# Attention of a fused kernel: transposes, projections and codes of the next head placed one by one between a group's other blocks

## The reference

```python
q_bits = (np.einsum('bhsd,dk->bhsk', q, proj) > 0)
k_bits = (np.einsum('bhsd,dk->bhsk', k, proj) > 0)
mask = q_bucket[:, :, :, None] == k_bucket[:, :, None, :]   # buckets: the 6 bits as a number
scores = np.where(mask, scale * np.matmul(q, k.transpose(0, 1, 3, 2)), -1000000000.0)
attn = softmax(scores)
x = (attn @ v) with the heads side by side                  # 1536 x 512
e_idx = np.argmax(x @ w_gate, axis=1)
x = gate * relu(x @ w1[e_idx]) @ w2[e_idx]                  # one expert per row
out = elu(x @ w_in) @ w_out
```

## Time and profile before

| | us |
|---|---|
| median of 3 runs | 815.64 |
| lowest, highest | 815.6, 816.53 |
| the profiled execution | 815.6 |
| its span, first to last instruction | 813.8 |
| attention's loop, from the first scores (10.60) to the first filler matmul behind it (284.58) | 274.0 |
| busy: TensorE matmuls, weight loads | 792.4, 658.3 |
| busy: VectorE, ScalarE, GpSimd | 453.5, 361.6, 340.4 |

### The profile page before, as it was taken

How to read it: one execution, slowest core, us unless ns; L and a number is a source line. 1 busy time by engine, 2 the same in 40 slices (tenths; PEclk the granted TensorE clock), 3 DMA queues, 4 the chain that set the end, 5 groups by cost and what they waited for, 6 DMA issues and landing times.

```text
span 813.8 us, 12942 instructions
## 1 busy us (share of the span) xinstructions
PE 792.4 (97%) x4389; PEld 658.3 (81%) x4389; DVE 453.5 (56%) x801; ACT 361.6 (44%) x684; POOL 340.4 (42%) x333
## 2 busy tenths in 40 slices
PE   7999999999999889999999999999999999999996
PEld 4777777777777668888888888889889989989985
DVE  5776767777777375454454454549516415613720
ACT  4677676776677413432234330037316405602710
POOL 4334343555556049977797785044210020000000
PEclk9999999999999999999999999999999999999999
DMA  5322232111200047675567660350010020000000
GB/s 151 98 66 76 66 92 94 40 50 42 67 12 18 13 129 277 233 239 199 179 229 236 194 215 18 105 194 0 18 61 2 1 61 17 1 14 27 1 14 26
DMA packets 40942, 72.68 MB, mean 89 GB/s; under 512 B 17904, under 2 KB 24304, under 8 KB 40880
## 3 DMA queue, kind: packets, MB, share of 16 engines
q10 hardware_dynamic: 10608, 33.69, 12.7%
q1 hardware_dynamic: 26832, 26.88, 10.5%
q0 software_dynamic: 3440, 11.28, 4.3%
HBM read 60.56 MB, written 11.28 MB: 88 GB/s over the span
## 4 chain that ended last, share of the span: by engine, by line
PE 92%; DVE 4%; ACT 2%; issue 1%; POOL 1%; DMA 0%; POOLq 0%; ACTq 0%; DVEq 0%
PE pair_t L1350 16%; PE pair_s L1248 13%; PE pair_t L1263 13%; PE pair_u L1118 8%; PE bank_b L1134 8%; PE pair_s L1300 7%; PE pair_u L1300 7%; PE pair_t L1107 4%; PE pair_s L1107 4%; PE bank_b L1145 2%; PE pair_u L1227 2%; PE bank_a L1085 2%; PE bank_a L1093 1%; PE bank_a L1074 1%; DVE g_lo L1054 1%
## 5 line engine op out<-in xcount | busy, mean ns | idle before, releaser
L432 POOL TENSOR_TENSOR w_part<-w_raw,w_part 128x1024 fp32r<-128x1024 f32 x80 | 190.0, 2406 | 51.7 <-ACT w_part L654 51.0
L654 ACT ACTIVATE w_part<-w_raw 128x1024 fp32r<-128x1024 f32 x72 | 73.5, 1055 | 183.8 <-PE pair_t L1263 149.1
L1350 PE MATMUL pair_t<-w_part,g_hi 128*128 128x512 f32 x384 | 118.8, 391 | 0.0
L1248 PE MATMUL pair_s<-w_part,xs_t 128*128 x456 | 108.8, 394 | 0.4 <-DVE xs_t L932 0.4
L1263 PE MATMUL pair_t<-w_part,hid_t 128*128 x456 | 109.0, 394 | 0.0
L563 POOL DMA_INDIRECT out<-o_sb,token x12 | 11.8, 986 | 216.4 <-DVE o_sb L1026 216.4
L1248 PEld LDWEIGHTS pair_s<-w_part,xs_t 128*128 128x128 f32 x456 | 84.2, 188 | 17.8 <-issue 0.9
L1263 PEld LDWEIGHTS pair_t<-w_part,hid_t 128*128 128x128 f32 x456 | 84.4, 189 | 16.8
L1118 PEld LDWEIGHTS pair_u<-first,exps 128*128 128x128 f32 x576 | 65.2, 141 | 27.7 <-ACT exps L614 19.2
L1118 PE MATMUL pair_u<-first,exps 128*128 128x128 f32 x576 | 83.9, 277 | 3.3 <-ACT exps_t L623 1.8
L1350 PEld LDWEIGHTS pair_t<-w_part,g_hi 128*128 128x128 f32 x384 | 71.7, 188 | 14.4
(11 more groups left out here) (196 smaller groups left out, 1214.7 us busy)
## 6 DMA issues: line engine op xcount, KB each, us to landing
w_raw<-in_moe_w ACTq DMA_DIRECT2D x48, 512.0 KB, 6.5
w_raw<-in_moe_w SPq DMA_DIRECT2D x16, 512.0 KB, 8.2
ys_sorted<-ys SPq DMA_DIRECT2D x19, 256.5 KB, 5.7
w_raw<-in_moe_w_in ACTq DMA_DIRECT2D x8, 512.0 KB, 7.1
w_raw<-in_moe_w_out ACTq DMA_DIRECT2D x8, 512.0 KB, 6.6
raw<-in_q SPq DMA_DIRECT2D x16, 192.0 KB, 2.4
raw<-in_k SPq DMA_DIRECT2D x16, 192.0 KB, 2.7
v_nat<-in_v SPq DMA_DIRECT2D x16, 192.0 KB, 2.5
```

Of the source, the lines that this page charges most:

```text
L432: pool.tensor_tensor(chunk_of(w_part, n, 1, c), w_raw[n % 2][c][:, :], chunk_of(w_part, n, 0, c).bitcast(F32), ALU.subtract).then_inc(s_wl ...
L654: act.activation(chunk_of(w_part, n, 0, c), w_raw[n % 2][c][:, :], ACT.Copy).then_inc(s_whi, 1)
L1248: mm = pe.matmul(pair_s[:, h, :], xs_t[:, xp, c * P:(c + 1) * P], w_part[:, bass.ds(par, 1), wp, a:a + 512], start=c == 0 and xp == 0 and ...
L1350: mm = pe.matmul(pair_t[:, t % 2, :], gp[:, f, j * P:(j + 1) * P], w_out_p[:, wp, f, :], start=f == 0 and m == 0, stop=f == FT - 1 and m == 2)
```

## The change

Nothing is added or taken away; the order in the queues changes on TensorE, VectorE and ScalarE. GpSimd's and SyncE's programs stay as they are.

- TensorE: both runs of scores now follow each other in every group. The chain of q starts one group earlier: `turn_qk(g + 1, 0)` stands in part 2 of head g, behind `last`; `project(g, 0)` in part 0 ahead of `times_v`, `code(g, 0)` behind it. For k: `turn_qk(g, 1)` in part 1 behind the scores, `project(g, 1)` behind `times_v`, `code(g, 1)` in part 2 behind the scores. `turn_qk(1, 0)` comes ahead of the loop.
- VectorE: `split_lo`, `sign` and `mask_even` move accordingly: part 0 has split_lo of q ahead of the maxima, sign behind them and the mask at the end; part 1 split_lo of k behind the maxima and sign at the end; part 2 the mask of k between the two maxima. `copy_t1(m_e + 1)` is written at the head of the next group. `inverse` and the weight cast move from part 0 to part 1.
- ScalarE: `copy_t0(m_e + 1)` is written at the head of the next group, `copy_rows` moves from part 2 to the next head's part 0, both exps come after the group's first copy, `mask_odd` of q ends part 0, that of k stands near the start of part 2, and `split_hi(g + 1, 0)` ends part 2.

```diff
--- before.py
+++ after.py
@@ -663,29 +663,31 @@
             act.activation(tiles(k_a, 0, 0)[0:D], tiles(k_b, 0, 1)[0:D].bitcast(F32), ACT.Copy).then_inc(s_cpa, 1)
             mask_odd(0, 0)
             mask_odd(0, 1)
+            split_hi(1, 0)
             for n in range(3, GROUPS):
                 g, part = n // 3, n % 3
                 m_s, m_e = 2 * (n - GROUP_S), 2 * (n - GROUP_E)
-                if g < HEADS and part >= 1:
-                    mask_odd(g, part - 1)
-                if part == 0 and m_s < J * HEADS:
-                    exp_rows(m_s)
+                if 0 <= m_e - 1 < J * HEADS - 1:
+                    copy_t0(m_e - 1)
+                if part == 0 and 3 <= g < HEADS + 2:
+                    copy_rows(g - 3)
+                if g < HEADS and part == 1:
+                    split_hi(g, 1)
+                if g < HEADS and part == 2:
+                    mask_odd(g, 1)
                 if 0 <= m_e < J * HEADS:
                     copy_t0(m_e)
-                if g < HEADS and part <= 1:
-                    split_hi(g, part)
-                if part >= 1 and m_s < J * HEADS:
+                if m_s < J * HEADS:
                     exp_rows(m_s)
-                if m_s < J * HEADS:
                     exp_rows(m_s + 1)
                 if n == 3 * HEADS + 3:
                     copy_t0(m_e + 1)
                 if g >= 2 and part <= 1:
                     copy_u(g - 2, part)
-                if 2 <= g < HEADS + 1 and part == 2:
-                    copy_rows(g - 2)
-                if 0 <= m_e < J * HEADS and n != 3 * HEADS + 3:
-                    copy_t0(m_e + 1)
+                if g < HEADS and part == 0:
+                    mask_odd(g, 0)
+                if g + 1 < HEADS and part == 2:
+                    split_hi(g + 1, 0)
             last_rows(HEADS - 1)
 
 
@@ -818,16 +820,24 @@
             for n in range(3, GROUPS):
                 g, part = n // 3, n % 3
                 m_s, m_e = 2 * (n - GROUP_S), 2 * (n - GROUP_E)
-                if g < HEADS and part >= 1:
-                    sign(g, part - 1)
-                    mask_even(g, part - 1)
+                if 0 <= m_e - 1 < J * HEADS:
+                    copy_t1(m_e - 1)
+                if g < HEADS and part == 0:
+                    split_lo(g, 0)
                 if m_s < J * HEADS:
                     row_max(m_s)
+                if g < HEADS and part == 2:
+                    mask_even(g, 1)
+                if m_s < J * HEADS:
                     row_max(m_s + 1)
+                if g < HEADS and part == 0:
+                    sign(g, 0)
+                if g < HEADS and part == 1:
+                    split_lo(g, 1)
                 if 0 <= m_e < J * HEADS:
                     copy_t1(m_e)
-                if g < HEADS and part <= 1:
-                    split_lo(g, part)
+                if g < HEADS and part == 0:
+                    mask_even(g, 0)
                 if n == 3:
                     dve.wait_ge(s_cst, 16)
                     dve.tensor_copy(last_w[:, :, 0:D],
@@ -836,15 +846,13 @@
                     dve.tensor_copy(tri_bf[:, :], cc("tri"))
                     dve.tensor_copy(ones_bf[:, :], cc("ones"))
                     dve.tensor_copy(iota_bf[:, :], cc("iota"))
-                if n == 3 * HEADS + 3:
-                    copy_t1(m_e + 1)
-                if part == 0 and g >= 2:
+                if part == 1 and g >= 2:
                     inverse(g - 2)
-                if part == 0 and 8 <= g < 8 + NCH:
+                if part == 1 and 8 <= g < 8 + NCH:
                     dve.wait_ge(s_wld[g - 8], 16)
                     dve.tensor_copy(chunk_of(w_part, 0, 0, g - 8), w_raw[0][g - 8][:, :]).then_inc(s_whi, 1)
-                if 0 <= m_e < J * HEADS and n != 3 * HEADS + 3:
-                    copy_t1(m_e + 1)
+                if g < HEADS and part == 1:
+                    sign(g, 1)
 
 
             then(dve.memset(onehot[:, TILES, :], 0.0))
@@ -1159,27 +1167,33 @@
             project(0, 1)
             code(0, 0)
             code(0, 1)
+            turn_qk(1, 0)
             for n in range(3, GROUPS):
                 g, part = n // 3, n % 3
                 m_s, m_e = 2 * (n - GROUP_S), 2 * (n - GROUP_E)
-                if g < HEADS and part >= 1:
-                    project(g, part - 1)
                 if m_s < J * HEADS:
                     scores(m_s)
-                if g < HEADS and part >= 1:
-                    code(g, part - 1)
-                if m_s < J * HEADS:
                     scores(m_s + 1)
+                if g < HEADS and part == 1:
+                    turn_qk(g, 1)
+                if g < HEADS and part == 2:
+                    code(g, 1)
                 if 0 <= m_e < J * HEADS:
                     turn_exps(m_e)
-                if g < HEADS and part <= 1:
-                    turn_qk(g, part)
+                if g < HEADS and part == 0:
+                    project(g, 0)
                 if n == 3 * HEADS + 3:
                     turn_exps(m_e + 1)
                 if g >= 2 and part <= 1:
                     times_v(g - 2, part)
                 if g >= 2 and part == 2:
                     last(g - 2)
+                if g < HEADS and part == 0:
+                    code(g, 0)
+                if g < HEADS and part == 1:
+                    project(g, 1)
+                if g + 1 < HEADS and part == 2:
+                    turn_qk(g + 1, 0)
                 if 0 <= m_e < J * HEADS and n != 3 * HEADS + 3:
                     turn_exps(m_e + 1)
```

## The result

| | before | after |
|---|---|---|
| median, us | 816.02 | 802.06 |
| lowest, highest | 815.6, 816.53 (4 runs) | 801.99, 802.19 (4 runs) |
| the profiled execution | 815.6 | 802.02 |
| its span | 813.8 | 800.2 |

The ratio is 0.9826, with a 95% interval of 0.9813 to 0.9839: 1.7% faster. The forecast was 802.5 us. Of the span, 13.6 us went. The medians differ by 14.0 us, 0.4 more than that, because two of the four executions of before took 0.8 to 0.9 us longer than the profiled one.

A forecast was written before the change was run, and what follows sets the result against it. TensorE's block starts were taken as the bound, 0.82 us per head lost to waits. 14 x (16.80 - 16.0) = 11.2, plus 1.4 and 0.5, is 13.1; 815.6 - 13.1 = 802.5 us, range 800.3 to 807.5.

The forecast's parts named there:

- head 1: First head: with the turn of q ahead of the loop, head 2 starts at 23.8, not 25.21; 1.4 us gained.
- end of attention: The 1.05 us wait for ScalarE's copy shrinks with the rows' copy put behind it; 0.5 us gained.
- Q: TensorE's three transposes of q or k, 0.33 us; one before part 2's last T covers VectorE's copy.
- C: TensorE's code matmul: costs 0.46 us where its columns need 0.175, so 0.29 lost to wait and late weight load.
- T: TensorE's six transposes of exps; the third group's last loses 0.24 us to the late copy of pair_u's upper half.
- The margin of 0.2: Part 2: VectorE's copy of pair_u's upper half ends at 4.0, TensorE wants it at 4.27; 0.2 us to spare.
- V: TensorE's exps times v, 2.09 us in parts 0 and 1.
- P: TensorE's projection; behind V in part 1 put at 0.62 us, bounds 0.53 to 0.81.
- the other estimate: Tiling-mode change drains TensorE: P and C behind V lose their early weight load, about 0.05 us each, 1.4 in all.
- S: One run of scores on TensorE, 4 matmuls; two alone take 1.48 us.
- The rest keeps up: Other engines deliver in time for TensorE's new order; thinnest margins in part 2, 0.2 us on VectorE, 0.45 on ScalarE.
- slower: Rival: part 2's chain of C, mask, second maximum, second exp delays the next S; 818.6 us at 1.6 longer; chance 0.05.

The follow-up runs named there:

- c_between: Changed kernel with the code matmul of k put back between the two runs of scores in part 2: 801.69 us.
- code_of_k_only: Kernel before with only the code of k moved behind both runs of scores, VectorE's mask of it between the maxima: 812.56 us.
- q_behind_t: Changed kernel with the turn of the next q behind, not in front of, the last turn of exps in part 2: 804.59 us.
- late_copy: Changed kernel with VectorE's weight cast of heads 8 to 15 moved ahead of the copy of pair_u in part 2: 806.21 us.
- late_exp: Changed kernel with ScalarE's copy of the rows back in part 2, ahead of its second exp: 806.54 us.
- codes_only: Kernel before with both codes behind both runs of scores and VectorE's mask between the maxima; projections and turns stay: 814.27 us.
- no_early_q: Changed kernel without the turn of head 1's q ahead of the loop; it follows the first two runs of scores: 804.65 us.

## Why the prediction came out right, point by point

| term | forecast | measured |
|---|---|---|
| part 0, part 1, part 2 | 5.59, 5.83, 4.51 (+0.07) | 5.59, 5.88, 4.53 |
| per head | 16.0 | 15.98 |
| 14 heads | 11.2 | 11.50 |
| head 1 | 1.4 | 1.66 |
| end of attention | 0.5 | 0.46 |
| sum | 13.1 | 13.6 |

- *Per head.* The measured 15.98 is a mean: a full head takes 16.00 (157.00 to 173.00), and head 15, which has no Q, 15.86.
- *C loses 0.29 us by having waited.* Right, and shown by c_between (no loss with the bits there) and code_of_k_only (0.32 back in one group). Both are about the C of k; that of q is shown by the kernel after alone, where it takes 0.17 behind V.
- *T loses 0.24 to a copy, and Q covers it.* Right, shown by q_behind_t and by head 15. The margin of 0.2 was right too: 0.18 by late_copy.
- *Blocks behind V.* P behind V takes 0.64 (161.66 to 162.30) against 0.62; C behind V shows its 0.17 alone. So the 0.07 us per head taken for both was 0.02, and the other estimate, 0.05 us for each of them and 1.4 us in all, did not come true. That a full head still came to 16.00 and not 15.95 is luck: two S take 1.50 instead of 1.48 in parts 1 and 2, and T, at 0.75 before V, 0.66 behind C and 0.58 elsewhere, takes 0.01 more than its term each time.
- *The rest keeps up.* Right, but more narrowly than I made it. On ScalarE the second exp with its accumulator is read was put at 4.8 from the group's start, and the margin of S at 0.45; late_exp leaves half of it. The chain's own rows in the kernel after say where it went. Counted from the group's start at 162.88, ScalarE's mask starts at 1.93 and the copy at 2.53 (forecast 1.95 and 2.45), but the first exp at 3.05 and not 2.8, because the copy takes 0.52 us to the next start and was given 0.35; the accumulator is read by 4.92. And S starts 0.15 us behind that read when it waits for it (154.64 and 154.79 in late_exp), not 0.06. So 5.31 - 4.92 - 0.15 = 0.24 us is left. The step of the prediction that was off is this one, and it did not decide. The *slower* rival would have decided at 1.25 us, and late_exp shows that its mechanism is real: 0.45 us more in the chain cost 4.5 us.
- *Head 1.* P starts at 12.07 (12.1 forecast) and C at 14.27 (14.3), the third group at 19.16 (19.4) and head 2 at 23.55 (23.8), so 0.25 us was gained between C and the third group. Since head 2 starts at 23.41 in the other profile of this kernel, half of that may be chance. T's wait for a copy is 0.48 where it was 0.70:

```profile
12.07 0.62 PE L1093 MATMUL bank_a<-q_b,proj_w 128*128 128x384 f32 x2
...
23.25 0.55 PE L1126 MATMUL pair_u<-first,exps 128*128 128x128 f32 x3 [0.48 <-DVE exps_t L795]
```

- *The end.* T waits 0.59 us for ScalarE's copy, where it waited 1.05:

```profile
261.98 0.85 PE L1126 MATMUL pair_u<-first,exps 128*128 128x128 f32 x6 [0.59 <-ACT exps_t L623]
```

- *What the prediction did not say.* It costed the whole and did not ask which part carries it. codes_only missed by 6 us for that reason: moving a step away from its wait helps only if the next step of the chain has room too.

## What to carry to other kernels

Where one engine is never idle for long, read its timeline from start to start and compare each block with the same block undisturbed; a wait of 0.2 us cost 0.3 here, since the next weights were not loaded ahead (behind C, and behind late_exp's wait; 0.05 more and not 0.1 in late_copy). A chain that hands work between engines is cured by putting other work of the busy engine between *each* pair of its steps: cured at one step alone, the wait moved to the next (0.13 us per head where 0.82 came from all). Then measure how thin the new margins are, by putting one instruction of known length in front of them.

## What the runs showed of the hardware that I had not expected

- In the first head TensorE's granted clock fell from 1.00 to 0.50 for 3.4 us in the profiles of three kernels (no_early_q, codes_only, code_of_k_only). From 12.0 to 15.2 us TensorE had been busy for 1.08 to 1.16 us of 3.2, and no single wait was longer than 2.12 us. A pair of S then took 0.64 us from start to start, not 0.35. The kernel before shows the same 1.10 us of work and the same 2.10 us wait as code_of_k_only in its profile, and keeps its clock. But this differs between executions of one kernel: of the 35 executions of before that ran beside the experiments, 17 at a mean granted clock of 0.997 to 0.999 took 815.31 to 816.25 us, and 18 at 0.992 to 0.996 took 816.42 to 818.69. All nine of the kernel after, busy for 1.79 us in that stretch in its profile, were at 0.998 or 0.999. So the clock costs the kernel before about 1 us in half of its executions and nothing in the profiled one. Where in those executions it fell, no profile shows, and what decides it stays open.
- The clock can fall in a later stage as well. In the profiled execution of late_copy it was at 0.50 from 290.8 to 294.2 us, behind attention, after TensorE had waited 1.24 and then 0.43 us; that execution took 808.15 us, the three others, at 0.998 and 0.999, 806.02 to 806.23.
- The same cast of 128x1024 on VectorE took 0.68 us in all eight heads of late_copy, with no instruction of GpSimd beside it. In the kernel before it took 0.87 us, in the kernel after 0.95 in seven heads, each time begun while a copy of GpSimd (0.51 us long) was under way, and in both it ended 0.55 us behind the end of that copy (131.23 and 131.78 in the kernel before, 129.39 and 129.94 in the kernel after). In the one head left of the kernel after (161.54) GpSimd's copy is recorded 0.04 us ahead of the cast, the cast took 0.65 and the copy 1.05 instead of 0.78. This looks as if the two engines took turns; no run was made to show it.
- A C between two S let the next S start 0.03 us later, and the time came back in that S (0.48 for its pair, not 0.35): single distances deceive, and only the sum over a few blocks can be read.
